# Six edits at the two ends of a kernel: key exponents behind K tiles, identity matmuls, a second numerator buffer, divided copies

## What is computed

```python
def phi(x):                                    # w_phi: 64 x 128
    proj = einsum('bhsd,df->bhsf', x, w_phi)
    proj = proj - max(abs(proj), axis=-1)
    return concatenate([exp(proj), exp(-proj)], axis=-1)
q_p, k_p = phi(q), phi(k)
kv  = einsum('bhsf,bhsd->bhfd', k_p, v)
z   = sum(k_p, axis=2)
att = einsum(q_p, kv) / (einsum(q_p, z) + 1e-6)         # x, 576 x 512 per batch

xk = mu_k * x + (1 - mu_k) * x_prev                     # x_prev: x shifted by one token
xr = mu_r * x + (1 - mu_r) * x_prev
y  = sigmoid(xr @ w_r) * (maximum(xk @ w_k, 0) ** 2 @ w_v)      # w_k 512x1024, w_v 1024x512

h  = maximum(y @ w_in, 0)
c  = 3-tap convolution of h along the tokens, by conv_w
out = (h * sigmoid(c)) @ w_out
```

## Time and profile before

| | |
|---|---|
| median of 3 runs | 1289.95 us (1288.88 to 1289.97) |
| profiled execution | 1286.36 us |
| its span | 1284.6 us |
| TensorE busy | 1265.4 us, 99% of the span |
| VectorE, ScalarE, GpSimd busy | 64%, 44%, 11% |
| granted TensorE clock, mean | 0.996 |

### The profile page before, as it was taken

The page is one execution under the profiler, slowest core; times in us unless marked ns, Lnnn a source line. Parts: engine busy times, 40 slices in busy tenths (PEclk is TensorE's granted clock), DMA queues, the critical chain, the costliest instruction groups (busy, mean ns, idle before and its releaser), DMA issues.

```text
span 1284.6 us, 23638 instructions
## 1 busy us (share of the span) xinstructions
PE 1265.4 (99%) x9506; PEld 1081.3 (84%) x9506; DVE 816.4 (64%) x1334; ACT 563.1 (44%) x1072; POOL 142.8 (11%) x137
## 2 busy tenths in 40 slices
PE   8889999999999999999999999999999999999998
PEld 6668887888788879788878878999899898898996
DVE  6788576576566766667657666546484583672852
ACT  4653634525434354353443544454344353352441
POOL 2512111102111211121111211000000000000000
PEclk8999999999999999999999999999999999999999
DMA  5512211221222222222131220422102102012001
GB/s 163 163 40 74 65 49 47 83 68 31 79 59 60 61 57 59 69 59 59 41 88 39 60 78 12 134 70 68 70 1 79 48 23 78 1 70 79 1 34 41
DMA packets 91540, 79.03 MB, mean 62 GB/s; under 512 B 61864, under 2 KB 70184, under 8 KB 90408
## 3 DMA queue, kind: packets, MB, share of 16 engines
q1 hardware_dynamic: 91272, 77.46, 19.9%
q10 hardware_dynamic: 160, 0.07, 0.0%
HBM read 58.21 MB, written 19.01 MB: 60 GB/s over the span
## 4 chain that ended last, share of the span: by engine, by line
PE 90%; DVE 3%; issue 3%; DMA 2%; ACT 1%; SPq 0%; ACTq 0%; DVEq 0%
PE psm L574 36%; PE ps L574 22%; PE psh L1197 6%; PE psh L1198 6%; PE psh L1196 6%; PE pso L1198 5%; PE pso L1196 5%; PE pso L1197 5%; PE ps L686 1%; DMA den<-den_scr 1%; ACT k_signs L826 1%; DMA den_scr<-den_cols 1%; DVE q_part L969 0%; DMA phi<-in_w_phi 0%; DVE mix L1034 0%
## 5 line engine op out<-in xcount | busy, mean ns | idle before, releaser
L574 PE MATMUL psm<-xy_hi,wk_hi 128*128 128x288 f32 x512 | 156.4, 306 | 6.6 <-DVE xy_lo L1053 3.9
L574 PE MATMUL psm<-k_hi,wv_hi 128*128 128x288 f32 x512 | 153.8, 300 | 0.0
L1198 PE MATMUL psh<-xy_hi,win_lo 128*128 128x288 f32 x512 | 151.3, 296 | 0.0
L1196 PE MATMUL psh<-xy_hi,win_hi 128*128 128x288 f32 x512 | 151.3, 296 | 0.0
L1197 PE MATMUL psh<-xy_lo,win_hi 128*128 128x288 f32 x512 | 151.3, 296 | 0.0
L574 PE MATMUL psm<-xy_lo,wk_hi 128*128 128x288 f32 x512 | 151.1, 295 | 0.0
L574 PE MATMUL psm<-k_lo,wv_hi 128*128 128x288 f32 x512 | 150.9, 295 | 0.0
L574 PE MATMUL psm<-k_hi,wv_lo 128*128 128x288 f32 x512 | 150.8, 295 | 0.0
L574 PE MATMUL psm<-xy_hi,wk_lo 128*128 128x288 f32 x512 | 150.7, 294 | 0.0
L1320 DVE SCALAR_TENSOR_TENSOR conv<-h,taps,conv 128x576 f32<-128x576 f32 x64 | 52.1, 814 | 138.8 <-ACT conv L1275 138.8
L562 POOL TENSOR_TENSOR z_pairs<-k_signs 128x512 f32<-128x512 f32 x56 | 73.2, 1307 | 601.7 <-ACT k_signs L826 597.7
(11 more groups left out here) (147 smaller groups left out, 2830.2 us busy)
## 6 DMA issues: line engine op xcount, KB each, us to landing
k_in<-in_k SPq DMA_DIRECT2D x32, 320.0 KB, 3.3
v_nat<-in_v SPq DMA_DIRECT2D x32, 320.0 KB, 3.6
q_in<-in_q SPq DMA_DIRECT2D x32, 288.0 KB, 3.1
y_scr<-y SPq DMA_DIRECT2D x64, 144.0 KB, 2.5
y<-y_scr SPq DMA_DIRECT2D x8, 1152.0 KB, 5.8
den<-den_scr SPq DMA_DIRECT2D x60, 144.0 KB, 3.0
out<-rows SPq DMA_DIRECT2D x32, 256.0 KB, 2.0
stage<-in_moe_w_in SPq DMA_DIRECT2D x4, 512.0 KB, 4.0
```

Source lines behind the costliest of these rows:

```text
L574: return nc.tensor.matmul(o, lhsT, rhs, start=first, stop=last, skip_group_check=True)
L1196: nc.tensor.matmul(o, wh, xh, start=first, stop=False, skip_group_check=True)
L1198: return nc.tensor.matmul(o, wl, xh, start=False, stop=last, skip_group_check=True)
```

## The change

It does six things.

1. In batch 0's attention: eight identity matmuls instead of seven at the very start, and a new step `WARM` with four identity matmuls, into a bank that VectorE has read by then, ahead of `KV0` of pair 0.
2. In batch 1's attention, pair 0's `EK` and `EL` leave their places ahead of the K tiles and come behind `K+` (0, 0) and `K+` (0, 1).
3. Pair 1's numerators of batch 0 go to `square`, a tile that is unused until the first K tile, and wait for nothing of VectorE.
4. `copy_wide` copies the first half of the denominators, the numerators, then the second half; the first halves can be inverted from then on, and the waits of TensorE for the banks count in halves.
5. In stage two VectorE copies output tiles 1 and 3, ScalarE 0, 2 and 4.
6. The fifth tile of the last two batches is computed, copied and stored in two halves of 256 columns.

```diff
-WARM_FIRST, WARM = 7, 6
+WARM_FIRST, WARM = 8, 4
-    steps = [("G", 0), ("F", 0), ("EK", 0), ("F", 1), ("QT", 0), ("KV0", 0), ("M", 0)] + hi()
+    steps = [("G", 0), ("F", 0), ("EK", 0), ("F", 1), ("QT", 0), ("WARM", 0), ("KV0", 0), ("M", 0)] + hi()
...
+    ("K+", 0, 0): [("EK", 0)],
+    ("K+", 0, 1): [("EL", 0)],
...
-            else:
+            elif step not in (("EK", 0), ("EL", 0)) or batch:
                 emit(step)
...
             if u:
-                eng.wait_ge(first_den, PAIRS - WIDE)
+                eng.wait_ge(first_den, 2 * (PAIRS - WIDE) + u - 2)
...
+            nc.scalar.activation(den_first[:, p - WIDE, 0:HALF], q_cols(1, p, a)[:, 0:HALF], ACT.Copy, bias=1e-6).then_inc(first_den, 1)
             nc.scalar.activation(num_first[:, p - WIDE, :], q_cols(0, p, a), ACT.Copy).then_inc(num_copied, 1)
-            nc.scalar.activation(den_first[:, p - WIDE, :], q_cols(1, p, a), ACT.Copy, bias=1e-6).then_inc(first_den, 1)
+            nc.scalar.activation(den_first[:, p - WIDE, HALF:S], q_cols(1, p, a)[:, HALF:S], ACT.Copy, bias=1e-6).then_inc(first_den, 1)
...
-            await_x(act, p, a)
-            nc.scalar.activation(num[:], q_cols(0, p, a), ACT.Copy).then_inc(num_copied, 1)
+            if (p, a) != (1, 0):
+                await_x(act, p, a)
+            nc.scalar.activation(numerator(p, a), q_cols(0, p, a), ACT.Copy).then_inc(num_copied, 1)
...
+    def last_columns(c):
+
+        halves = slice(0, DM // 2), slice(DM // 2, DM)
+        return halves if c == TWOS - 1 else (slice(0, DM),)
...
-                for j in range(FT):
-                    last = out_part(0, 4, j)
-                last.then_inc(out_done, 1)
+                for n, cols in enumerate(last_columns(c)):
+                    for j in range(FT):
+                        last = out_part(0, 4, j, cols, n)
+                    last.then_inc(out_done, 1)
...
-            for t in range(4 + half):
+            for t in range(0, 4 + half, 2):
                 copy_rows(c, half, t)
...
+        def copy_rows(c, half, t):
+            dve.wait_ge(out_done, token_tiles(c, half, t + 1))
+
+            if c > 0:
+                dve.wait_ge(stored[t], c * 32 + 16 * half)
+            elif half:
+                dve.wait_ge(stored[t], 16)
+            nc.vector.tensor_scalar(rows[:, t, :], o_bank(t), 0.5, None, ALU.mult).then_inc(odd_rows, 1)
...
+            for t in (1, 3):
+                copy_rows(c, half, t)
```

More of the change, by code:

```diff
@@ L392, in await_q_psum, with numerator @@
             eng.wait_ge(num_copied, PAIRS - 1)
-            eng.wait_ge(first_den, PAIRS - 1 - WIDE)
+            eng.wait_ge(first_den, 2 * (PAIRS - 1 - WIDE))
         else:
             await_(eng, num_copied, PAIRS, a, p)
+    def numerator(p, a):
+        return square[:].rearrange("p i s -> p (i s)") if (p, a) == (1, 0) else num[:]
     def two(sbuf_cols):
@@ L999, in divide @@
             await_(dve, r_mixed, 2 * XT, a, 0)
-            nc.vector.tensor_tensor(x[:, p, 1:1 + S], num[:], den[:], ALU.mult).then_inc(x_ready, 1)
+            nc.vector.tensor_tensor(x[:, p, 1:1 + S], numerator(p, a), den[:], ALU.mult).then_inc(x_ready, 1)
         def divide_half(n, p):
             cols, own = slice(HALF * n, HALF * n + HALF), p - WIDE
-            dve.wait_ge(first_den, own + 1)
+            dve.wait_ge(first_den, 2 * own + n + 1)
             nc.vector.reciprocal(den_first[:, own, cols], den_first[:, own, cols]).then_inc(first_inverse, 1)
@@ L1152, in token_tiles, with await_rows, await_all_rows @@
         return c * TILES + (4 * half + n)
+    def await_rows(eng, c, half, t):
+        eng.wait_ge((even_rows, odd_rows)[t % 2], c * (4 + (t + 1) % 2) + 2 * half + t // 2 + 1)
+    def await_all_rows(eng, c, half):
+        eng.wait_ge(even_rows, 5 * c + 2 * half)
+        eng.wait_ge(odd_rows, 4 * c + 2 * half)
+    def last_columns(c):
+        halves = slice(0, DM // 2), slice(DM // 2, DM)
+        return halves if c == TWOS - 1 else (slice(0, DM),)
     def y_tiles(c, half, n):
@@ L1162, in two, with o_bank @@
         return cols.rearrange("p (b s) -> p b s", s=HALF)
-    def o_bank(t):
-        return pso[:, t, :] if t < 4 else psh[:, 1, 1, :]
+    def o_bank(t, n=0):
+        return pso[:, t, :] if t < 4 else psh[:, 1, 1 - n, :]
     def sync(sp):
@@ L1170, in store @@
             for t in range(4):
-                sp.wait_ge(rows_ready, token_tiles(c, half, t + 1))
+                await_rows(sp, c, half, t)
                 sp.dma_start(out[c * 2 + half][P * t:P * t + P, :], rows[:, t, :]).then_inc(stored[t], 16)
             if half:
-                sp.wait_ge(rows_ready, token_tiles(c, 1, 5))
-                sp.dma_start(out[c * 2 + 1][4 * P:S, :], rows[0:TAIL, 4, :]).then_inc(stored[4], 16)
-                sp.dma_start(out[c * 2][4 * P:S, :], rows[TAIL:P, 4, :]).then_inc(stored[4], 16)
+                for n, cols in enumerate(last_columns(c)):
+                    await_rows(sp, c, 1, 4 + 2 * n)
+                    sp.dma_start(out[c * 2 + 1][4 * P:S, cols], rows[0:TAIL, 4, cols]).then_inc(stored[4], 16)
+                    sp.dma_start(out[c * 2][4 * P:S, cols], rows[TAIL:P, 4, cols]).then_inc(stored[4], 16)
         def load_y(b):
@@ L1188, in sync @@
         store(TWOS - 1, 1)
-        for s in stored:
+        for s in stored[0:4]:
             sp.wait_ge(s, 16 * B)
+        sp.wait_ge(stored[4], 16 * B + 32)
     def tensor(pe):
@@ L1198, in three, with out_part @@
             return nc.tensor.matmul(o, wl, xh, start=False, stop=last, skip_group_check=True)
-        def out_part(at, t, j):
+        def out_part(at, t, j, cols=slice(0, DM), n=0):
             tok = slice(at + P * t, at + P * t + P)
-            return three(o_bank(t), (g_hi[:, j, tok], g_lo[:, j, tok]), (wout_hi[:, j, :], wout_lo[:, j, :]), j == 0, j == FT - 1)
+            return three(o_bank(t, n)[:, cols], (g_hi[:, j, tok], g_lo[:, j, tok]), (wout_hi[:, j, cols], wout_lo[:, j, cols]), j == 0, j == FT - 1)
         def batch(c, half):
@@ L1221, in batch @@
             else:
-                pe.wait_ge(rows_ready, token_tiles(c, half, 0))
+                await_all_rows(pe, c, half)
             for j in range(FT):
@@ L1253, in copy_rows @@
                 act.wait_ge(stored[t], 16)
-            nc.scalar.activation(rows[:, t, :], o_bank(t), ACT.Copy, scale=0.5).then_inc(rows_ready, 1)
+            for n, cols in enumerate(last_columns(c) if t == 4 else (slice(0, DM),)):
+                act.wait_ge(out_done, token_tiles(c, half, t + 1 + n))
+                nc.scalar.activation(rows[:, t, cols], o_bank(t, n)[:, cols], ACT.Copy, scale=0.5).then_inc(even_rows, 1)
         act.wait_ge(taps_loaded, 48)
```

4 lines of the change are left out of this document (2 added, 2 removed).

## The result

The changed kernel takes 1280.37 us (median of 5 executions, 1279.83 to 1283.55), the kernel before on the same chip 1289.97 (1288.88 to 1292.05): a ratio of 0.9929 with a 95% interval of 0.9914 to 0.9945. The two profiled executions, 1286.36 and 1279.83 us, are only 6.5 apart. So the traces hold two thirds of the gain, and the rest has to be looked for in what the one profiled execution of the kernel before did not show.

The account below looks back on a forecast made before the run. TensorE, busy 99% of the span, was taken as the bound, with gains only from idle time, a slow clock and the end; −1.8 − 1.9 + 0.3 − 0.2 − 2.0 + 0.8 + 0 − 0.1 = −4.9 gave 1285.0 us, range 1282.7 to 1287.6.

Parts of the forecast that it names:

- the term for pair 1's numerators, −1.9: Batch 0: ScalarE copies pair 1's numerators without waiting for VectorE's `x`, so pair 3's projections start sooner; 1.9 us gained.
- the first rival: The clock falls in the first batch all the same, leaving −3.1 us, 1286.9 us; chance 28%.
- my 4.9: The forecast's whole gain over all terms, −4.9 us, from the median 1289.95 to 1285.0 us.
- The clock in the first batch, −1.8: Four added matmuls ahead of `KV0` keep the clock at 2.4 GHz, speeding pair 0's denominators and numerators; 1.8 us gained.
- a rival with 8%: The eighth matmul at the start wakes TensorE earlier, so the first projections gain another 1 us, 1284.0 us; chance 8%.
- the 4.94 us: Pair 0's denominators and numerators, read as 4.94 us at 1.2 GHz and expected to take 3.25 at the high clock.
- The copies of pairs 2 and 3, +0.3 and −0.2: Three copies for two: 0.3 us later exponents and `KV1` of pair 3, 0.2 gained by pair 3's earlier first half.
- the exponents, −2.0: Batch 1: later key exponents move GpSimd's sums off VectorE's last quarter of x, cutting TensorE's 2.7 us wait by 2.0.
- The chain: VectorE's operations for the last quarter of x ahead of `K+`, forecast to shrink from 4.31 us to 2.2.
- The `relu`s, +0.8: Exponents between the first K tiles delay ScalarE's `relu`, so TensorE's fifth and sixth tiles wait; 0.8 us lost.
- Row copies and the last tile, −0.1: Stage two: row copies moved to VectorE worth 0, the last tile in halves with a shorter final copy; 0.1 us gained.

Follow-up runs that it names:

- e3: The kernel before with eight identity matmuls at the very start instead of seven, nothing else: 1288.57 us, ratio 0.9994.
- e6: The changed kernel with pair 1's numerators put back to wait for x of pair 0: 1283.56 us, ratio 0.9951.
- e9: The kernel before with identity matmuls filling its two largest stalls, five ahead of pair 3's projections and eleven ahead of the first `K+`: 1284.89 us, ratio 0.9969.
- e10: The kernel before with pair 1's numerators in a tile of their own, nothing else: 1284.43 us, ratio 0.9967.
- e11: The kernel before with the key exponents of batch 1's pair 0 behind the first two `K+` tiles, nothing else: 1286.80 us, ratio 0.9999.
- e2: The changed kernel without the step `WARM` (four identity matmuls ahead of `KV0`): 1280.93 us, ratio 0.9932.
- e5: The changed kernel with `EK` and `EL` of batch 1's pair 0 back ahead of the first K tiles: 1282.72 us, ratio 0.9948.
- e8: The changed kernel with the copies of pairs 2 and 3 in their old form, numerators then whole denominators: 1281.34 us, ratio 0.9936.
- e1: The changed kernel with seven identity matmuls at the very start instead of eight: 1279.84 us, ratio 0.9930.
- e4: The kernel before with both clock edits, eight identity matmuls at the start and the step `WARM` with four: 1287.48 us, ratio 0.9982.
- e7: The changed kernel with the whole stage two of the kernel before, row copies on ScalarE and last tile in one piece: 1280.66 us, ratio 0.9929.
- e15: The changed kernel with the fifth output tile of the last batches in one piece: 1279.54 us, ratio 0.9944.
- e16: The changed kernel itself, unchanged, run again on the fourth chip for comparison: 1280.50 us, ratio 0.9944.
- e12: The changed kernel with four more identity matmuls ahead of the first `PICK` of batch 0: 1278.53 us, ratio 0.9919.
- e13: e12 with the two key exponents one K tile later, behind `K+` (0, 1) and `K+` (0, 2): 1279.11 us, ratio 0.9923.
- e14: The kernel before with identity matmuls in every thin place (those of e4, e9 and e12 together), its waits all kept: 1285.05 us, ratio 0.9980.

## Why the prediction was wrong

**The step that failed** is the term for pair 1's numerators, −1.9. It is priced as idle time alone, with the clock behind the stall at nothing, and the ground for that is the sentence against the first rival: "the other stalls of the first 80 us, one of 2.7 us, were followed by no fall". That sentence was read from one execution, with a mean clock of 0.996. In half of the 82 executions a further 10 to 14 us are spent at 1.2 GHz, and the traces of e3 and e6 show where: behind the 1.3 to 1.7 us stall for pair 1's numerators near 44 us. Those executions are 1289.76 − 1285.43 = 4.3 us slower. I had also added the 3.6 us between the profiled execution and the median unexamined, as if they were a constant that both kernels have. They are not: the changed kernel's profiled execution is 0.5 us below its median. The difference, 3.1 us, is most of what the forecast misses.

**What shows the cause.** Filling the stalls with matmuls, without freeing any work to start earlier, gives 4.4 us (e9). Removing the stall of the numerators alone gives 3.7 (e10); putting it back costs 3.2 and brings the stay back in one execution of six, the profiled one (e6), so that no kernel without the unfilled stall has an execution at 0.992 or less, and the stall alone is not enough for the long stay. Shortening the stall at the K tiles alone gives nothing measurable (e11). Like for like, executions with one stay of 8 to 10 us in both kernels, the change is worth 1285.43 − 1280.93 = 4.5 us, taking the median of the nine such executions of the changed kernel (5.1 with the 1280.37 of the first five), against my 4.9. So the sum was about right for executions without the long stay.

**The clock in the first batch, −1.8.** In the two profiled executions the size was right by luck, and the reason wrong. `WARM` did not hold the clock in this one: `PICK` waits 1.11 us for `max_blocks` behind thin 65-column matmuls, and 0.50 follows. The 2.1 us of lead came from waking earlier: the key projections at 6.12 take 1.58 us, against 2.80 before. I had set that aside as a rival with 8%, by the eighth matmul.

In other executions `WARM` does seem to hold the clock longer. In all five traces without it in which TensorE had woken by then (the kernel before, e2, e3, e9, e11) the clock falls between 16.6 and 18.0 us. With it, and without the four matmuls ahead of `PICK`, it falls between 18.7 and 20.2 us in four traces (the changed kernel, e5, e6, e8) and not at all there in five (e1, e4, e7, e15, e16). That is a count over few traces and not a test. For the waking, some 2 us here, the same holds: with seven matmuls TensorE woke after 10 us in three of five traces, with eight in one of thirteen (e3), so the eighth may have a share, though e3 and e1 show none in the median. When TensorE wakes differs between executions of the same kernel, and what decides it stays open. My reading of the 4.94 us was loose as well: the clock came back at 28.1 us, so they were not all at 1.2 GHz.

What does hold the clock is four more matmuls in the gap before `PICK` (e12 and e13, twelve executions of twelve at 0.999 or 1.0, against two of eleven of the changed kernel). In e12 pair 1's `KV0` starts at 25.61 in the trace instead of 27.29, and the median is 1.8 us lower, measured apart and with overlapping intervals; the narrow spread of the times speaks for it as well.

**Pair 1's numerators, −1.9.** In the traces the lead grows from 2.1 to 4.0 by pair 2's denominators, so the idle time was sized right; the clock behind it was left out, as told above.

**The copies of pairs 2 and 3, +0.3 and −0.2, and the exponents, −2.0.** Together −1.9; the lead grows by 2.2 at the first `K+`. The copies' +0.3 is not seen, and e8 puts both within the noise. The chain came out as summed, operation by operation.

**The `relu`s, +0.8.** It was 1.0 (lead 6.2, then 5.2), at the two tiles named, though in pieces of 0.26 and less beside slower starts. The whole of this part, undone in e5, is worth 2.3 us, of which a stay at 0.50 of 3.4 us is a share; I had 1.2 net. The sums come in time: TensorE waits for none of them, and not for `max_blocks` before the K tiles are done.

**Row copies and the last tile, −0.1.** The row copies cost nothing, as said; there is no wait of TensorE in stage two. The last tile gives −0.6 in the trace (4.4 us from the last matmul's start to the end of the span before, 3.8 after) and 0.7 between e15 and e16: I counted the copy, which gives 0.22 of it, and not the shorter last matmul (0.13) and what lies behind the copy (0.3), where the smaller store is. Both lie under the spread of the medians.

The lead of 6.6 us at the end is then 2.1 + 1.9 + 2.2 − 1.0, the 0.7 near 800 us that no edit explains, and 0.7 at the end; with the drift between them this is 1.7 more than my 4.9.

**Still open**: which executions the clock falls in, behind the same stall. e14, with the large stalls of the first 80 us filled, should have been the best of the versions of the kernel before and was not. In its trace the added matmuls delay nothing at the two large stalls, since TensorE still waits 1.27 us for `num` and 0.34 for `xy_lo` behind them; 1.7 us are lost by the stay at 51.6 and as much by the longer waits for `relu`, for which the runs show no reason. Three executions of the kernel before took 1289.2 to 1290.5 us at a clock of 0.999. A late waking, such as in e10's trace, does not lower that mean, but it costs that trace only some 2 us by 31 us, which is not enough.

## What to carry to other kernels

A profiled execution that is faster than the median by more than the spread of a few runs is a finding, not an offset: compare the granted clock of several executions before a sum is made against one trace. A stall of 1 to 2 us between thin matmuls costs its own length and, in some executions, a stretch at half clock behind it (here some 4 us), so that filling it with matmuls nobody reads can gain as much as removing it. Price such a stall with both ends, and fill the ones that can't be removed.

## What the hardware showed that I had not expected

- The clock fell after waits of only 1.1 us (changed kernel, 18.6), 1.3 (e6), 1.57 (e14) and 1.66 us (e3), each amid 65-column or few matmuls, and behind waits of the same size it did not: 1.26 us in the earlier trace rows, and 1.06 before `PICK` in e1's trace. The Trainium skill, "TensorE: Matmul & The Clock Gate", section "HAM oscillation — how this bites in real kernels", puts a fall down to idle gaps that are longer than any of these waits; by that rule none of them would have cost any clock. The rows contradict it here.
- Stays at 0.50 that the traces hold had lengths of 3.4, 6.8, 10.2 and 13.7 us.
- In e10's trace TensorE woke only at about 28 us. The granted clock reads 1.00 in every window from the start, but the query projections of pair 1 take 3.15 us instead of 1.79 and the first `KV0` 4.21 instead of 2.28. So a granted clock of 1.00 at the very start said nothing there; the durations did.
